# Split order in an expert's first tile: both hidden halves ahead of the next expert's weight blocks

## The chip, the cores and the metric

One core of one Trainium2 chip runs the whole program in one launch. The metric is the device time in microseconds of that core, as the median over executions. TensorE is PE in the rows, with its weight loads as PEld; VectorE is DVE, ScalarE is ACT, GpSimd is POOL and SyncE is SP.

## The reference, cut to what matters

Three stages in a row: attention with pooled queries, a gated mixer, and a mixture of eight experts. The change is in the third one. For every token, one expert `e` is chosen:

```
h = np.maximum(x[b, s] @ w1[e], 0.0)      # 512 -> 1024
out[b, s] = p[e] * (h @ w2[e])            # 1024 -> 512
```

There are 4 x 576 = 2304 tokens. The products are to be exact to about single precision.

## The kernel before, in words

The first two stages end with the tokens sorted by expert in DRAM (`sorted_dram`) and a small table of counts. Function `experts` (line 1376) then works through the experts that have tokens, one after the other, in tiles of 128 tokens. In this run six experts are in use, with 2, 7, 1, 5, 5 and 2 tiles, 22 in all. They are called e0 to e5 here, and the tiles g0 to g21; the first tiles of e0 to e4 are g0, g2, g9, g10 and g15. The numbers of tiles are read by the engines at run time.

Every fp32 product is made of three passes over a high and a low part: ACT rounds a block to its high part (a copy to `F32R`), and DVE or POOL subtracts it from the original to have the low part. This is what "split" means below. It is done for activations and for weights.

One tile on PE (lines 1571 to 1587):

- `first(par, 0, ...)`: 12 matmuls, columns 0 to 511 of the first product into `first_ps[0]`; then 4 matmuls of the second half into `first_ps[1]`.
- `turn_h(g, 0)`: four transposes of the first half of `hidden` into `ht_ps[0]`. They wait for `relu_a`, the ReLU on ACT (L1653).
- the other 8 matmuls of `first(par, 1, ...)`.
- a wait for `ht_lo`, then 6 matmuls of `second` (L1556), `turn_h(g, 1)` (which waits for `relu_b`, the ReLU on DVE, L1724), 6 more, and `turn_x(g + 1)`: four transposes of the next tile's rows into `xt_ps` (L1533), which wait for the rows' DMA.
- a second wait for `ht_lo`, and the last 12 matmuls of `second`. The next tile begins with a wait for `xt_lo`.

ACT rounds `ht_ps[0]`, `ht_ps[1]` (`h_high`, L1609) and `xt_ps` (`x_high`, L1605). DVE makes the low parts (`h_low`, L1679; `x_low`, L1672), and then, for the tile's end, `index` (L1732), `result` (L1734, from `second_ps`) and the next tile's `tag` (L1685). POOL stores `result` by an indirect DMA (L1510).

In an expert's first tile the same engines also split the next expert's weights. w1 has four pieces: ACT rounds them (L1619), DVE subtracts (L1692). w2 has four pieces: ACT rounds them (L1625), POOL subtracts (L1477). Nothing schedules this but the order of the program: each engine has one stream, and `tile` on ACT (line 1651) and on DVE (line 1720) has `split(...)` written between the steps of the tile. Weights of the expert after that are loaded by DMA when their buffer is free: w1 from ACT's queue (L1629), w2 in two halves from POOL's (L1486). An expert's first matmul waits for all four `w1_lo` pieces (line 1569).

Before the change, in an expert's first tile, ACT runs: ReLU, `h_high(g, 0)`, three pieces of w1, `h_high(g, 1)`, `x_high(g + 1)`, the fourth piece of w1, four pieces of w2, and then the ReLU of the second tile. DVE runs: `h_low(g, 0)`, ReLU, one piece, `h_low(g, 1)`, `x_low(g + 1)`, one piece, `index`, `result`, `tag`, the last two pieces, and then the `h_low(g, 0)` of the second tile.

Of the kernel before, what the change touches and what calls it, by code (L numbers as in the profile page):

```python
# [1375 lines left out]
def experts(nc, ctx, sorted_dram, counts, consts, w1, w2, out, stage, first_loaded, first_mark):  # L1376
# [55 lines left out]
    def entry(eng, what, place):  # L1432
        return eng.value_load(counts[0:1, bass.ds(place + what * LIST, 1)], min_val=0, max_val=LIMITS[what])  # L1433
# [8 lines left out]
    with nc.Block() as block:  # L1442
# [147 lines left out]
        def tiles(eng, n, before, tile, split, next_in_use):  # L1590

            with eng.If(n > 0):
                tile(before, next_in_use)
                with eng.If(n > 1):
                    with eng.Fori(1, n) as i:
                        tile(before + i, None)
            with eng.If(n < 1):
                with eng.If(next_in_use > 0):
                    split(range(2 * PIECES))

        @block.scalar
        def _(act):
            def x_high(g):
                act.wait_ge(s["x_turned"], g + 2)
                nc.scalar.copy(xt_h[:].rearrange("p k r -> p (k r)"), xt_ps[:]).then_inc(s["xt_hi"], 1)  # L1605

            def h_high(g, half):
                act.wait_ge(s["h_turned"], 2 * g + half + 1)
                nc.scalar.copy(ht_h[:, 4 * half:4 * half + 4].rearrange("p k r -> p (k r)"), ht_ps[half][:]  # L1609
                               ).then_inc(s["ht_hi"], 1)  # L1610

            def high(e, j, par, pieces):

                for piece in pieces:
                    k = piece % PIECES
                    if piece < PIECES:
                        if k == 0:
                            act.wait_ge(w1_loaded[par], 16 * (j + 1))
                        nc.scalar.copy(w1_h[par][:, k], w1_raw[par][:, k]).then_inc(s["w1_hi"], 1)  # L1619
                    else:  # L1620
                        if isinstance(e, int):
                            act.wait_ge(piece_loaded[k], 16)
                        elif k % 2 == 0:
                            act.wait_ge(half_loaded[k // 2], 16 * e)
                        nc.scalar.copy(w2_h[par][:, 2 * k:2 * k + 2], w2_raw[:, 2 * k:2 * k + 2]  # L1625
                                       ).then_inc(s["w2_hi"], 1)

            def load1(e, par):
                act.dma_start(w1_raw[par], w1_d[entry(act, EXPERT, e)]).then_inc(w1_loaded[par], 16)  # L1629

            high(0, 0, 0, range(PIECES))
            for k in range(PIECES):
                act.dma_start(w2_raw[:, 2 * k:2 * k + 2], w2_d[0][:, 2 * k:2 * k + 2]
                              ).then_inc(piece_loaded[k], 16)
            x_high(0)
            high(0, 0, 0, range(PIECES, 2 * PIECES))
            with act.If(entry(act, IN_USE, 1) > 0):
                load1(1, 1)

            def place(j, par):  # L1640
                e = 2 * j + par
                with act.If(entry(act, IN_USE, e + 2) > 0):
                    act.wait_ge(s["w1_lo"], PIECES * e + PIECES)
                    load1(e + 2, par)
                n, before = (entry(act, what, e) for what in (TILES, BEFORE))
                next_in_use = entry(act, IN_USE, e + 1)

                def split(pieces):
                    high(e + 1, j + par, 1 - par, pieces)

                def tile(g, splits):
                    act.wait_ge(s["first_done"], 2 * g + 1)
                    nc.scalar.activation(hidden[:, 0:FHALF], first_ps[0][:], ACT.Relu).then_inc(s["relu_a"], 1)  # L1653
                    h_high(g, 0)
                    if splits is not None:
                        with act.If(splits > 0):
                            split(range(3))
                    h_high(g, 1)
                    x_high(g + 1)
                    if splits is not None:  # L1660
                        with act.If(splits > 0):
                            split(range(3, 2 * PIECES))

                tiles(act, n, before, tile, split, next_in_use)

            places(act, place)

        @block.vector
        def _(dve):
            def x_low(g):  # L1670
                dve.wait_ge(s["xt_hi"], g + 1)
                nc.vector.tensor_tensor(xt_l[:].rearrange("p k r -> p (k r)"), xt_ps[:],  # L1672
                                        xt_h[:].rearrange("p k r -> p (k r)").bitcast(F32), ALU.subtract
                                        ).then_inc(s["xt_lo"], 1)

            def h_low(g, half):
                part = slice(4 * half, 4 * half + 4)
                dve.wait_ge(s["ht_hi"], 2 * g + half + 1)
                nc.vector.tensor_tensor(ht_l[:, part].rearrange("p k r -> p (k r)"), ht_ps[half][:],  # L1679
                                        ht_h[:, part].rearrange("p k r -> p (k r)").bitcast(F32), ALU.subtract  # L1680
                                        ).then_inc(s["ht_lo"], 1)

            def take_tag(g):
                dve.wait_ge(s["rows_loaded"], 16 * (g + 1))
                nc.vector.tensor_copy(tag[:], rows_in[:, DM:ROW]).then_inc(s["tag_taken"], 1)  # L1685

            def low(e, par, pieces):

                for k in pieces:
                    if k < PIECES:  # L1690
                        dve.wait_ge(s["w1_hi"], PIECES * e + k + 1)
                        nc.vector.tensor_tensor(w1_l[par][:, k], w1_raw[par][:, k],  # L1692
                                                w1_h[par][:, k].bitcast(F32), ALU.subtract
                                                ).then_inc(s["w1_lo"], 1)


            dve.sem_inc(s["tag_taken"], 1)
            dve.sem_inc(s["result_ready"], 1)
            low(0, 0, range(PIECES))
            take_tag(0)  # L1700
            x_low(0)
            for k in range(PIECES):
                part = slice(2 * k, 2 * k + 2)
                dve.wait_ge(s["w2_hi"], k + 1)
                nc.vector.tensor_tensor(w2_l[0][:, part], w2_raw[:, part], w2_h[0][:, part].bitcast(F32),
                                        ALU.subtract).then_inc(s["w2_lo"], 1)

            def place(j, par):
                e = 2 * j + par
                n, before = (entry(dve, what, e) for what in (TILES, BEFORE))  # L1710
                next_in_use = entry(dve, IN_USE, e + 1)

                def split(pieces):
                    low(e + 1, 1 - par, pieces)

                def maybe_split(splits, pieces):
                    if splits is not None:
                        with dve.If(splits > 0):
                            split(pieces)

                def tile(g, splits):
                    h_low(g, 0)
                    dve.wait_ge(s["first_done"], 2 * g + 2)
                    nc.vector.tensor_scalar(hidden[:, FHALF:F2], first_ps[1][:], 0.0, None, ALU.max  # L1724
                                            ).then_inc(s["relu_b"], 1)
                    maybe_split(splits, range(1))
                    h_low(g, 1)
                    x_low(g + 1)
                    maybe_split(splits, range(1, 2))
                    dve.wait_ge(s["tag_taken"], g + 2)  # L1730
                    dve.wait_ge(s["stored"], 16 * g + 16)
                    nc.vector.tensor_copy(index[:], tag[:, 1:2].bitcast(U32)).then_inc(s["result_ready"], 1)  # L1732
                    dve.wait_ge(s["second_done"], g + 1)
                    nc.vector.tensor_scalar(result[:], second_ps[:], tag[:, 0:1], None, ALU.mult  # L1734
                                            ).then_inc(s["result_ready"], 1)
                    dve.wait_ge(s["result_ready"], 2 * g + 3)
                    take_tag(g + 1)
                    maybe_split(splits, range(2, PIECES))

                tiles(dve, n, before, tile, split, next_in_use)  # L1740

            places(dve, place)
# [43 lines left out]
```

## Time and profile before

| | before |
|---|---|
| median of 3 runs | 1269.45 us (1269.32 to 1272.0) |
| the profiled execution, its own time | 1270.8 us |
| its span in the trace | 1269.1 us |
| mean granted clock of TensorE | 0.959 |
| busy: PE, DVE, ACT, POOL | 1172.0, 785.4, 567.6, 537.0 us |
| busy share: PE, DVE, ACT, POOL | 92%, 62%, 45%, 42% |

The experts run from about 952 us to the end. An ordinary tile there takes 12.50 us, in which PE never stops; first tiles and the tiles behind them take longer. A timeline row gives the start in us from the span's start, the duration in us, and in brackets how long the engine had been idle before, with what released it. The start and the duration of neighbouring rows may overlap a little, since an engine begins an instruction before the last one has drained: ACT's casts of 128x1024 last 1.05 us each but follow each other every 0.95 us.

### The profile page before, as it was taken

How to read it: one execution, taken by the hardware profiler on the slowest of the kernel's cores; microseconds unless marked ns; L12 is line 12 of the kernel's file. 1: busy time of each engine (PE TensorE's matmuls, PEld its weight loads, DVE VectorE, ACT ScalarE, POOL GpSimd, SP SyncE). 2: the span in 40 equal slices, each digit the busy share in tenths (PEclk: the TensorE clock that was granted, in tenths of full speed). 3: DMA queues.
4: the chain of work that ended last, by engine and by line, in shares of the span. 5: the costliest groups of instructions: out<-in, count | busy, mean ns of one | idle time of the engine just before them, and what ended most of it. 6: DMA issues, size and time to landing. Idle time of an engine off the chain costs nothing. (4 is left out here: it accounts for less than half of the span.)

```text
span 1269.1 us, 23908 instructions
## 1 busy us (share of the span) xinstructions
PE 1172.0 (92%) x7459; PEld 1053.0 (83%) x7460; DVE 785.4 (62%) x1501; ACT 567.6 (45%) x1022; POOL 537.0 (42%) x597
## 2 busy tenths in 40 slices
PE   6999999999999999997889999999825999799997
PEld 5999999999999999996777989889714778577786
DVE  4888988888888888986532643526134532453532
ACT  4666666666666666663412223222105411341411
POOL 6777777777777777753100010100111520350400
PEclk9999999999999999998899999999856999899999
DMA  5121221212121221101301020120137531350110
GB/s 193 40 65 56 65 65 46 65 56 65 37 65 56 65 65 48 45 9 52 118 1 38 1 75 0 37 83 0 37 104 282 173 108 50 114 203 33 42 33 30
DMA packets 49579, 86.40 MB, mean 68 GB/s; under 512 B 8142, under 2 KB 20558, under 8 KB 49552
## 3 DMA queue, kind: packets, MB, share of 16 engines
q1 hardware_dynamic: 39264, 52.49, 13.2%
q0 software_dynamic: 5984, 19.95, 4.7%
q10 hardware_dynamic: 4304, 13.64, 3.0%
q8 instruction: 13, 0.21, 0.1%
q14 instruction: 14, 0.11, 0.0%
HBM read 69.77 MB, written 17.33 MB: 69 GB/s over the span
## 5 line engine op out<-in xcount | busy, mean ns | idle before, releaser
L618 DVE TENSOR_SCALAR_CACHE_REDUCE probs<-scores 128x1152 f32<-128x1152 f32 x144 | 195.5, 1358 | 61.0 <-PE scores L472 60.0
L472 PE MATMUL scores<-k_t,q_t 128*128 128x384 f32 x960 | 201.7, 347 | 1.3 <-DVE probs L618 1.3
L570 ACT ACTIVATE probs<-probs,neg_max 128x1152 f32<-128x1152 f32 x144 | 181.8, 1263 | 0.0
L594 ACT CAST pt_h<-ring 128x384 fp32r<-128x384 f32 x288 | 139.0, 483 | 73.6 <-PE ring L479 67.8
L495 PE MATMUL acc<-pt_h,v_parts 128*128 128x256 f32 (+1 forms) x576 | 169.3, 316 | 0.6 <-DVE pt_l L684 0.6
L479 PE MATMUL ring<-consts,probs 128*128 128x128 f32 x1296 | 165.4, 273 | 0.7 <-DVE pt_l L684 0.7
L472 PEld LDWEIGHTS scores<-k_t,q_t 128*128 128x128 f32 x960 | 160.7, 189 | 2.2 <-DVE probs L618 2.1
L495 PE MATMUL acc<-pt_l,v_parts 128*128 128x256 f32 (+1 forms) x576 | 157.2, 295 | 0.0
L328 POOL TENSOR_TENSOR pt_l<-mid,pt_h 128x384 fp32r<-128x384 f32 x144 | 145.5, 1010 | 12.0
L479 PEld LDWEIGHTS ring<-consts,probs 128*128 128x128 f32 x1296 | 146.2, 141 | 2.5 <-DVE pt_l L684 1.8
L684 DVE TENSOR_TENSOR pt_l<-ring,pt_h 128x384 fp32r<-128x384 f32 x288 | 145.8, 548 | 0.0
L863 POOL DMA_INDIRECT sorted_tokens<-y,slot x20 | 19.2, 962 | 294.0 <-DVE y L1311 289.1
L325 POOL TENSOR_SCALAR pt_h<-mid 128x384 fp32r<-128x384 f32 x144 | 74.2, 515 | 131.7 <-DVE mid L681 129.9
L495 PEld LDWEIGHTS acc<-pt_h,v_parts 128*128 128x128 f32 x576 | 108.6, 189 | 0.9 <-ACT out_t L577 0.8
L495 PEld LDWEIGHTS acc<-pt_l,v_parts 128*128 128x128 f32 x576 | 109.1, 189 | 0.0
L1679 DVE TENSOR_TENSOR ht_l<-ht_ps,ht_h 128x512 fp32r<-128x512 f32 x44 | 30.4, 691 | 108.1 <-ACT ht_h L1609 108.1
L1510 POOL DMA_INDIRECT out<-result,index x22 | 23.2, 1053 | 159.5 <-DVE result L1734 158.1
L1548 PE MATMUL first_ps<-w_h,xt_h 128*128 128x512 f32 x176 | 72.2, 410 | 10.3 <-DVE w_l L1692 7.0
L681 DVE COPY mid<-ring 128x384 f32<-128x384 f32 x144 | 79.6, 553 | 1.8 <-PE ring L479 1.8
L1556 PE MATMUL second_ps<-w_h,ht_h 128*128 128x512 f32 x176 | 74.0, 421 | 5.9 <-DVE ht_l L1679 5.9
L1548 PE MATMUL first_ps<-w_l,xt_h 128*128 128x512 f32 x176 | 72.9, 414 | 0.0
L1477 POOL TENSOR_TENSOR w_l<-w_raw,w_h 128x1024 fp32r<-128x1024 f32 x20 | 51.7, 2613 | 48.6 <-ACT w_h L1625 48.5
(195 smaller groups left out, 2530.3 us busy)
## 6 DMA issues: line engine op xcount, KB each, us to landing
w_raw<-moe_w POOLq DMA_DIRECT2D x10, 1024.0 KB, 6.2
k_nat<-k SPq DMA_DIRECT2D x32, 288.0 KB, 2.8
v_nat<-v SPq DMA_DIRECT2D x32, 288.0 KB, 2.8
q_nat<-q SPq DMA_DIRECT2D x32, 256.0 KB, 2.9
w_raw<-moe_w ACTq DMA_DIRECT2D x3, 2048.0 KB, 11.0
rows_in<-sorted_tokens SPq DMA_DIRECT2D x23, 257.0 KB, 2.6
x_in<-x_heads SPq DMA_DIRECT2D x18, 256.0 KB, 3.3
x_heads<-x_pair SPq DMA_DIRECT2D x16, 256.0 KB, 2.4
```

The costliest lines, as they stand in the source:

```text
L325: nc.gpsimd.tensor_scalar(out, src, 1.0, 1.0, ALU.mult, ALU.mult).then_inc(signal, 1)
L328: nc.gpsimd.tensor_tensor(out, src, high_part.bitcast(F32), ALU.subtract).then_inc(signal, 1)
L472: mm = nc.tensor.matmul(scores[:, c, 0:CK], q_t[par][:, side, t * P:(t + 1) * P], k_t[par][:, c * CK:(c + 1) * CK], start=(i == 0), stop=( ...
L479: mm = nc.tensor.transpose(ring[c][:, i * P:(i + 1) * P], probs[n % 3][:, c, i * P:(i + 1) * P], ident)
L495: mm = nc.tensor.matmul(acc[:, 0:b - a], v_parts[par][:, kt], part[:, kt, a:b], start=(kt == 0 and part is pt_h), stop=(kt == KT - 1 and p ...
L570: nc.scalar.activation(probs[n % 3][:], probs[n % 3][:], ACT.Exp, bias=neg_max[:, n % 3:n % 3 + 1], scale=-1.0, accum_out=row_sum[:, n:n + ...
L594: nc.scalar.copy(pt_h[:, 3 * c:3 * c + 3, n * P:(n + 1) * P], ring[c][:, 0:CK].rearrange("p (i r) -> p i r", i=3)).then_inc(s["high_done"], 1)
L618: nc.vector.tensor_scalar(probs[n % 3][:], scores[:, :, 0:CK], -0.5 * DH ** -0.5, None, ALU.mult, ALU.min, accum_out=neg_max[:, n % 3:n % ...
L681: nc.vector.tensor_copy(mid[n % 3][:], ring[1][:, 0:CK]).then_inc(s["mid_done"], 1)
L684: nc.vector.tensor_tensor(pt_l[:, 3 * c:3 * c + 3, cols], ring[c][:, 0:CK].rearrange("p (i r) -> p i r", i=3), pt_h[:, 3 * c:3 * c + 3, co ...
L1548: mm = nc.tensor.matmul(first_ps[half][:], a[:, k], w[:, k, cols], start=(i == 0), stop=(i == 3 * KD - 1))
L1556: mm = nc.tensor.matmul(second_ps[:], a[:, k], w[:, k], start=(k == 0 and n == 0), stop=(k == K2 - 1 and n == 2))
```

## The change

In `tile`, ACT's `h_high(g, 1)` is moved ahead of `split(range(3))`, and DVE's `h_low(g, 1)` ahead of `split(range(1))`. In tiles without a split nothing differs.

```diff
@@ scalar, tile @@
                     h_high(g, 0)
+                    h_high(g, 1)
                     if splits is not None:
                         with act.If(splits > 0):
                             split(range(3))
-                    h_high(g, 1)
                     x_high(g + 1)
@@ vector, tile @@
+                    h_low(g, 1)
                     maybe_split(splits, range(1))
-                    h_low(g, 1)
                     x_low(g + 1)
```

ACT, an expert's first tile, from the ReLU on (L1653 the ReLU, L1609 `h_high`, L1619 the pieces of w1 of the next expert, L1605 `x_high`):

```order
 L1653 ACTIVATE hidden<-first_ps 128x512
 L1609 CAST ht_h<-ht_ps 128x512
-L1656 COMPARE_AND_BRANCH
+L1608 REGISTER_ALU
+L1609 CAST ht_h<-ht_ps 128x512
+L1657 COMPARE_AND_BRANCH
 L1618 ISA
 L1619 CAST w_h<-w_raw 128x1024 x3
-L1656 UNCONDITIONAL_BRANCH
-L1608 REGISTER_ALU
-L1609 CAST ht_h<-ht_ps 128x512
```

The second cast of `ht_ps` with its wait now stands ahead of three casts of weights instead of behind them.

DVE, the same tile, from its ReLU on (L1724 the ReLU, L1679 `h_low`, L1692 a piece of w1's low part, L1672 `x_low`):

```order
 L1724 TENSOR_SCALAR hidden<-first_ps 128x512
+L1679 TENSOR_TENSOR ht_l<-ht_ps,ht_h 128x512
 L1718 COMPARE_AND_BRANCH
 L1691 ISA
 L1692 TENSOR_TENSOR w_l<-w_raw,w_h 128x1024
 L1718 UNCONDITIONAL_BRANCH
-L1679 TENSOR_TENSOR ht_l<-ht_ps,ht_h 128x512
 L1671 REGISTER_ALU
 L1672 TENSOR_TENSOR xt_l<-xt_ps,xt_h 128x512
```

The second subtraction now stands ahead of the one piece of weights instead of behind it. The streams of PE, POOL and SP are the same as before, with their DMAs, and no instruction is added or taken away on any engine.

## Rows read from the trace of the kernel before

**Rows 1.** Waits from 950 us to the end: total us, times, longest us.
```profile
PE second_ps L1556 <- DVE ht_l L1679: 5.9, 4, 1.9
PE first_ps L1548 <- DVE w_l L1692: 7.0, 1, 7.0
```
**Rows 2.** Timeline of ACT, e3's first tile: start, us, what, [idle before].
```profile
1112.28 0.59 ACT L1609 CAST ht_h<-ht_ps 128x512 fp32r<-128x512 f32 x1 [0.77 <-PE ht_ps L1540]
1112.77 2.94 ACT L1619 CAST w_h<-stage 128x1024 fp32r<-128x1024 f32 x3
1115.98 0.59 ACT L1609 CAST ht_h<-ht_ps 128x512 fp32r<-128x512 f32 x1 [0.27 <-PE ht_ps L1540]
1117.81 0.59 ACT L1605 CAST xt_h<-xt_ps 128x512 fp32r<-128x512 f32 x1 [1.25 <-PE xt_ps L1533]
...
1121.40 2.00 ACT L1625 CAST w_h<-w_raw 128x1024 fp32r<-128x1024 f32 x2 [0.16 <-DMA w_raw<-moe_w]
1123.41 0.60 ACT L1653 ACTIVATE hidden<-first_ps 128x512 f32<-128x512 f32 x1
```
**Rows 3.** Timeline of DVE, e3's first tile from `x_low` to the second tile's `h_low`.
```profile
1118.43 0.69 DVE L1672 TENSOR_TENSOR xt_l<-xt_ps,xt_h 128x512 fp32r<-128x512 f32 x1 [1.14 <-ACT xt_h L1605]
1119.04 1.22 DVE L1692 TENSOR_TENSOR w_l<-stage,w_h 128x1024 fp32r<-128x1024 f32 x1
...
1120.62 0.75 DVE L1734 TENSOR_SCALAR result<-second_ps,tag 128x512 f32<-128x512 f32 x1 [0.30 <-PE second_ps L1556]
1121.49 1.33 DVE L1685 COPY tag<-rows_in 128x2 f32<-128x2 f32 x1
1122.74 4.55 DVE L1692 TENSOR_TENSOR w_l<-stage,w_h 128x1024 fp32r<-128x1024 f32 x2
1127.21 0.68 DVE L1679 TENSOR_TENSOR ht_l<-ht_ps,ht_h 128x512 fp32r<-128x512 f32 x1
```
**Rows 4.** Timeline of POOL, the same stretch.
```profile
1120.38 5.83 POOL L1477 TENSOR_TENSOR w_l<-w_raw,w_h 128x1024 fp32r<-128x1024 f32 x2 [6.30 <-ACT w_h L1625]
```
**Rows 5.** Timeline of PE, e3's second tile: three of its rows.
```profile
1120.41 0.40 PE L1548 MATMUL first_ps<-w_h,xt_h 128*128 128x512 f32 x1
...
1124.14 0.60 PE L1540 MATMUL ht_ps<-consts,hidden 128*128 128x128 f32 x4
...
1127.94 0.50 PE L1556 MATMUL second_ps<-w_h,ht_h 128*128 128x512 f32 x1 [1.33 <-DVE ht_l L1679]
```
**Rows 6.** Timeline of ACT, e1's first tile: `h_high(g, 1)` and `x_high`.
```profile
1003.85 0.59 ACT L1609 CAST ht_h<-ht_ps 128x512 fp32r<-128x512 f32 x1 [0.27 <-PE ht_ps L1540]
1006.70 0.59 ACT L1605 CAST xt_h<-xt_ps 128x512 fp32r<-128x512 f32 x1 [2.27 <-PE xt_ps L1533]
```
**Rows 7.** Timeline of ACT, e0's two tiles.
```profile
974.35 2.94 ACT L1619 CAST w_h<-w_raw 128x1024 fp32r<-128x1024 f32 x3 [2.63 <-DMA w_raw<-moe_w]
977.20 0.57 ACT L1609 CAST ht_h<-ht_ps 128x512 fp32r<-128x512 f32 x1
...
982.92 2.00 ACT L1625 CAST w_h<-w_raw 128x1024 fp32r<-128x1024 f32 x2 [1.82 <-DMA w_raw<-moe_w]
985.99 0.60 ACT L1653 ACTIVATE hidden<-first_ps 128x512 f32<-128x512 f32 x1 [1.06 <-PE first_ps L1548]
```
**Rows 8.** Timeline of PE, e0: transposes, the matmul that waited, the second tile's first.
```profile
974.20 0.60 PE L1540 MATMUL ht_ps<-consts,hidden 128*128 128x128 f32 x4
...
978.55 0.50 PE L1556 MATMUL second_ps<-w_h,ht_h 128*128 128x512 f32 x1 [1.93 <-DVE ht_l L1679]
...
982.76 0.63 PE L1548 MATMUL first_ps<-w_h,xt_h 128*128 128x512 f32 x1
```
**Rows 9.** PE by stretches: length, PE busy (matmuls), granted clock, DMA share, GB/s.
```profile
980.00:983.00 3.00, 3.00 (x8) 0.50 0.64 246
...
1015.00:1018.00 3.00, 1.67 (x8) 1.00 0.24 19
...
1106.30:1109.60 3.30, 3.22 (x8) 0.50 0.70 199
```

## Prediction

> **What bounds the kernel now.** I read the waits of the experts' stage first, then the timelines of ACT, DVE, POOL and PE around one first tile, then the granted clock. The waits show that PE sets the pace: in the last 319 us it waits for a low part of `hidden` four times, 5.9 us in all, and once for a low part of w1, 7.0 us [rows 1]. The four are 1.93 us in e0's first tile [rows 8] and 1.33 us in the second tile of e1, e3 and e4, of which one is shown [rows 5]. So the question for each of the five first tiles (g0, g2, g9, g10, g15) is whether the second half of `hidden` is what PE waits for, and what the moved step pushes back.
>
> It is what PE waits for in e0 only. There three weight casts had waited for their DMA until 974.35, and the cast of `ht_ps[1]` came at 977.20 [rows 7], though its transposes, begun at 974.20, last 0.60 us [rows 8]. In the other four the three casts fit into the time in which ACT would wait for the transposes anyway: in e3 they run from 1112.77 to 1115.71, ACT is then idle for 0.27 us, and the cast of `ht_ps[1]` starts at 1115.98, when PE is ready [rows 2]. e1 shows the same 0.27 [rows 6]. The move takes nothing from these.
>
> **The change, step by step, in e3's first tile.** With the new order ACT stands still from the end of its first cast (1112.87) to 1115.98. The three weight casts follow that cast: they start 0.48 us behind it (as 1112.77 behind 1112.28, rows 2) at 1116.46 and take 3 x 0.95, so `xt_h` starts at 1119.31. Before, it started at 1117.81: 1.50 us later. The fourth w1 cast and the first w2 cast follow at once in both orders, so they are 1.50 later too. This is the price of the edit: 2.85 us of weight casts moved out of a cover of 3.1 us into a place where 1.25 us of idle time [rows 2] was free.
>
> Who waits for that. (a) PE's next tile needs `xt_lo`: DVE starts 0.62 behind ACT and takes 0.69, so 1119.31 + 1.31 = 1120.62, against PE's start at 1120.41 [rows 5]: some 0.25 us, not lasting, since a later wait is longer. (b) The ReLU of the second tile stands behind the w2 casts. 1119.31 + 0.48 + 0.95 + 4 x 0.95 = 1124.54 instead of 1123.41, 1.13 later, and PE's transposes follow it directly [rows 2, 5]. (c) DVE: `x_low`, the second piece and `index` are 1.50 later. `result` had 0.30 us of idle time before it [rows 3], so it is 1.20 later. (d) POOL's first subtraction waits for ACT's first w2 cast, so it goes from 1120.38 to 1121.88, 1.50 later [rows 4].
>
> DVE's last two weight pieces decide, since the second tile's `ht_l` stands behind them, and PE had already waited 1.33 us for it: no slack is left there. Alone a piece takes 1.22 us (the row at 1119.04); beside POOL two take 4.55, and the tag copy ended 2.44 us behind POOL's start (1121.49 + 1.33 against 1120.38) [rows 3, 4]. e1's and e4's do so too. I read it as DVE and POOL taking turns, so that the chain hangs on POOL's start, and take 1.50 us for e3; without that link it would be 1.20. The Trainium skill, "SBUF — State Buffer", says of the port pair that DVE and GpSimd share that it is an exclusive lock held for the whole instruction, the other one fully blocked. By that rule each such shift is 1.50 us and the sum for e2, e3 and e4 is 4.5 us; if the two only slowed each other down, it would be 3.6.
>
> The other tiles. **e4** is e3 again: +1.50. **e2** has one tile, and PE waits 7.0 us for the last w1 piece [rows 1], which is the same chain on DVE: +1.50. **e1**: the rows of the next tile came late, ACT had 2.27 us of idle time before `x_high` [rows 6], and 1003.85 + 0.48 + 2.85 = 1007.18 is only 0.48 behind 1006.70: +0.48.
>
> **e0** gains. The cast of `ht_ps[1]` can start at about 974.84, `ht_l` ends 1.31 later at 976.15, and PE, whose idle time began at 978.55 - 1.93 = 976.62 [rows 8], goes on without it. `xt_h` then starts at 974.84 + 0.48 + 2.85 = 978.17, 0.49 later than before; PE's second tile can start at about 979.55, 3.2 us earlier than the 982.76 of before [rows 8]. But its transposes of `hidden` wait for a ReLU that stands behind two w2 casts on ACT, which waited for their DMA until 982.92 [rows 7]. The DMA's issue does not move. They end at 984.92, so the ReLU gains 985.99 - 984.9 = 1.1 us and no more. PE, ahead by then, waits some 2.2 us for it.
>
> The clock comes in here. Before, it was at 0.50 of full speed (the 1.2 GHz level) in the 3 us from 980 on, right behind the idle 1.93 us, while in the stretch of e1's 1.33 us, from 1015 to 1018, it stayed at 1.00 [rows 9]. A fall cost some eight matmuls (x8 in 3.0 us, rows 9) of about 0.427 us instead of 0.233 (e3's twelve and four from 1120.41 to 1124.14, rows 5, 3.73 / 16): 1.55 us. The 2.2 us wait is longer than the one that was followed by a fall, so I count one: e0 comes to -1.1 + 1.55 = about +0.4 against this trace. In e0 before, half of the fall was hidden behind the same ReLU.
>
> The second tiles of e1, e3 and e4 then have waits of about 1.6, 1.7 and 1.7 us for `ht_l`, where they had 1.33 (1.33 + 1.50 - 1.13 = 1.70). That lies between the row that kept its clock and the row that lost it. Unknown, so bounded: no fall, 0; a fall in all three, +4.6 us. A gain is excluded, since none of these tiles is at the lower clock now. The middle of the two rows is 1.63, with two waits just above and one at it; I count one fall of three, +1.5. After e2 PE restarts at 0.50 as it does now [rows 9] for a few us; I take no difference, with a bound of +0.7 and -0.7 (about half of a fall).
>
> Nothing is issued more or less. SP's row loads wait for `tag`, and move with it by up to 1.5 us, but the transposes that need them come a tile later. POOL's stores and w2 loads move with their chain.
>
> **Sum.** 0.48 + 3 x 1.50 + 0.4 + 1.5 = 6.9 us. Against the profiled execution's own 1270.8 that is 1277.7. The median of the three runs, 1269.45, lies 1.35 below it, so I set the forecast at 1269.45 + 6.9 = **1276.4 us**, 0.54% slower.
>
> **The rivals.**
>
> *The clock holds everywhere in the second tiles.* The sum is 5.4 with e0's fall, 3.9 without: 1273.3 to 1274.9. For it speaks that 1.33 us of idle time was kept three times of three. It is still slower, and I hold it with the forecast as one mechanism with two sizes: forecast (one or two falls) 0.50, this one 0.26.
>
> *The clock falls in all three second tiles*, and the restart after e2 is longer: 6.9 + 3.1 + 0.7 = 10.7, 1280.2. Each wait alone is below 1.93. Chance 0.12.
>
> *The delay of ACT is mostly free.* If the next rows came as late in e2, e3 and e4 as in e1, each shift would be 0.48 and not 1.50: 4 x 0.48 + 0.4 = 2.3, 1271.8, within the noise. Against it: e3 waits 1.25 us for the transposes themselves and not for a DMA [rows 2]. Chance 0.09.
>
> *Faster: only e0 counts.* If ACT's queue went past the waiting cast to the weight casts behind it, the order of the program would not matter in e1 to e4, and e0 would keep its 1.1 us: 1268.3, and with the clock's fall avoided and the DMA earlier by more than 2 us, up to 3.2: 1266.2. It decides from the point where `xt_h` in e2 to e4 is late by less than 0.2 us. Against it: ACT's rows stand in program order everywhere, and in e0 the cast of `ht_ps[1]` did wait behind casts that waited for a DMA [rows 7]. Chance 0.03.
>
> **How the numbers follow.** A measurement of this kernel can tell about 0.2%, 2.5 us, from no change. The two clock sizes and the full fall are slower by more than that: 0.50 + 0.26 + 0.12 = 0.88. The mostly free case is the same, 0.09, and the last one faster, 0.03. The range goes from 1272.4, the case with no fall at all less the 0.9 us by which DVE's shifts may be smaller, to 1280.2, the full fall. It leaves out the last two cases, 0.12, and what lies beyond the bounds.
>
> **What would show it.** ACT's cast of `ht_ps[1]` directly behind the first one in the row order, with 3.1 us of idle time before it in e1 to e4; `xt_h` 3.33 us behind the moved cast instead of 1.83; POOL's first subtraction and `ht_l` of the second tile both 1.5 us later against PE's first transposes; PE's wait before it 1.6 to 1.7 us plus some 0.8 us before the transposes; PE's wait in front of e3 8.5 us instead of 7.0; no wait for `ht_l` in e0's first tile, but one of about 2.2 us before the second tile's transposes. I am wrong if PE's second tiles of e3 and e4 start their `second` matmuls by less than 1 us later, or if e0 gains more than 1.5 us.

## The result, and the profile after

| | before | after |
|---|---|---|
| median | 1269.48 us (1264.08 to 1272.0, 12 runs) | 1276.46 us (1273.23 to 1278.67, 12 runs) |
| the profiled execution, its own time | 1270.8 us | 1276.51 us |
| its span | 1269.1 us | 1274.9 us |
| mean granted clock | 0.959 | 0.957 |

The ratio is 1.0056, with a 95% interval of 1.0043 to 1.0069: the change makes the kernel 7.0 us slower (5.5 to 8.8). The two profiled executions differ by 5.7 us in their own times.

Waits from 950 us to the end, after (total us, times, longest us):

```profile
PE first_ps L1548 <- DVE w_l L1692: 8.4, 1, 8.4
PE second_ps L1556 <- DVE ht_l L1679: 5.2, 3, 1.7
PE ht_ps L1540 <- ACT hidden L1653: 3.4, 4, 1.9
```

Against [rows 1]: of the four waits for a low part of `hidden`, e0's of 1.93 us is gone, and the three others grew from 1.33 to 1.73. The wait in front of e3 grew from 7.0 to 8.4. The third row is new against this trace of before. PE waits for the ReLU four times: 1.85 us in e0's second tile, and 0.50 in those of e1, e3 and e4.

ACT in e3's first tile, after (answers to [rows 2]):

```profile
1114.96 0.58 ACT L1609 CAST ht_h<-ht_ps 128x512 fp32r<-128x512 f32 x1 [0.77 <-PE ht_ps L1540]
1118.66 0.58 ACT L1609 CAST ht_h<-ht_ps 128x512 fp32r<-128x512 f32 x1 [3.12 <-PE ht_ps L1540]
1119.15 2.95 ACT L1619 CAST w_h<-stage 128x1024 fp32r<-128x1024 f32 x3
1122.00 0.58 ACT L1605 CAST xt_h<-xt_ps 128x512 fp32r<-128x512 f32 x1
1122.47 1.05 ACT L1619 CAST w_h<-stage 128x1024 fp32r<-128x1024 f32 x1
1123.42 3.89 ACT L1625 CAST w_h<-w_raw 128x1024 fp32r<-128x1024 f32 x4
1127.22 0.59 ACT L1653 ACTIVATE hidden<-first_ps 128x512 f32<-128x512 f32 x1
```

From one cast of `ht_ps` to the other ACT does nothing for 3.12 us, and the idle time before `xt_h` is gone. `xt_h` starts 1122.00 - 1118.66 = 3.34 us behind the moved cast, where it was 1.83. The ReLU starts 8.56 us behind it, where it was 7.43.

DVE, the same stretch, after (answers to [rows 3]):

```profile
1122.61 0.69 DVE L1672 TENSOR_TENSOR xt_l<-xt_ps,xt_h 128x512 fp32r<-128x512 f32 x1 [1.15 <-ACT xt_h L1605]
1123.22 1.21 DVE L1692 TENSOR_TENSOR w_l<-stage,w_h 128x1024 fp32r<-128x1024 f32 x1
...
1124.42 0.74 DVE L1734 TENSOR_SCALAR result<-second_ps,tag 128x512 f32<-128x512 f32 x1
1125.28 1.70 DVE L1685 COPY tag<-rows_in 128x2 f32<-128x2 f32 x1
1126.90 4.55 DVE L1692 TENSOR_TENSOR w_l<-stage,w_h 128x1024 fp32r<-128x1024 f32 x2
1131.37 0.68 DVE L1679 TENSOR_TENSOR ht_l<-ht_ps,ht_h 128x512 fp32r<-128x512 f32 x1
```

POOL, after (answers to [rows 4]):

```profile
1124.55 5.81 POOL L1477 TENSOR_TENSOR w_l<-w_raw,w_h 128x1024 fp32r<-128x1024 f32 x2 [8.38 <-ACT w_h L1625]
```

PE in e3's second tile, after (answers to [rows 5]):

```profile
1123.36 0.50 PE L1548 MATMUL first_ps<-w_h,xt_h 128*128 128x512 f32 x1
...
1127.86 0.65 PE L1540 MATMUL ht_ps<-consts,hidden 128*128 128x128 f32 x4 [0.50 <-ACT hidden L1653]
1132.10 0.50 PE L1556 MATMUL second_ps<-w_h,ht_h 128*128 128x512 f32 x1 [1.73 <-DVE ht_l L1679]
```

Taken from the moved cast, POOL's first subtraction starts at 5.89, where it was 1120.38 - 1115.98 = 4.40: 1.49 later. `result` is 1.12 later (5.76 against 4.64), yet the second tile's `ht_l` is 1.48 later (12.71 against 11.23). So DVE lost 0.36 us more between the two rows. The difference sits in the tag copy, which took 1.70 us where it took 1.33. It ended 1126.98 - 1124.55 = 2.43 us behind POOL's start; before it was 2.44. DVE reached the copy earlier against POOL and was let in no sooner.

e0, ACT after (answers to [rows 7]):

```profile
974.68 0.58 ACT L1609 CAST ht_h<-ht_ps 128x512 fp32r<-128x512 f32 x1 [3.12 <-PE ht_ps L1540]
...
982.68 1.99 ACT L1625 CAST w_h<-w_raw 128x1024 fp32r<-128x1024 f32 x2 [1.25 <-DMA w_raw<-moe_w]
984.58 0.59 ACT L1653 ACTIVATE hidden<-first_ps 128x512 f32<-128x512 f32 x1
```

and PE after (answers to [rows 8]):

```profile
985.23 0.66 PE L1540 MATMUL ht_ps<-consts,hidden 128*128 128x128 f32 x4 [1.85 <-ACT hidden L1653]
```

PE by stretches, after (length, PE busy, granted clock, DMA share, GB/s; answers to [rows 9]):

```profile
980.00:983.00 3.00, 3.00 (x15) 1.00 0.42 160
986.80:990.00 3.20, 3.20 (x9) 0.50 0.41 101
1130.00:1133.00 3.00, 1.27 (x6) 1.00 0.28 18
```

The fall of the clock moved from behind the wait at 976.6 to behind the one at 983.4. In e3's second tile 1.73 us of waiting left it at full speed.

So that traces can be compared, I use the ReLU's starts (L1653), from an expert's first tile to its third, and for e2 from its one tile to e3's first:

| us | e0 | e1 | e2 | e3 | e4 |
|---|---|---|---|---|---|
| before, first trace | 29.02 | 27.63 | 21.22 | 26.61 | 26.61 |
| after, first trace | 29.44 | 28.09 | 23.27 | 28.09 | 28.10 |
| difference | +0.42 | +0.46 | +2.05 | +1.48 | +1.49 |

The differences sum to 5.9 us, which is all that the two spans differ by (5.8).

### The profile page after: what moved, and what is told of

Its sections match the earlier page's. It is cut to its first block and busy times, and to the rows that moved or that the text cites. A ratio compares the mean times of both kernels' runs of the same rounds, so it can differ in the third digit from the quotient of the medians.

```text
span 1274.9 us, 23908 instructions
## 1 busy us (share of the span) xinstructions
PE 1174.4 (92%) x7459; PEld 1053.0 (83%) x7460; DVE 788.9 (62%) x1501; ACT 566.3 (44%) x1022; POOL 537.0 (42%) x597
## 5 line engine op out<-in xcount | busy, mean ns | idle before, releaser
L325 POOL TENSOR_SCALAR pt_h<-mid 128x384 fp32r<-128x384 f32 x144 | 74.0, 514 | 132.4 <-DVE mid L681 130.7
L1679 DVE TENSOR_TENSOR ht_l<-ht_ps,ht_h 128x512 fp32r<-128x512 f32 x44 | 30.3, 690 | 114.0 <-ACT ht_h L1609 114.0
```

The costliest lines, as they stand in the source:

```text
L325: nc.gpsimd.tensor_scalar(out, src, 1.0, 1.0, ALU.mult, ALU.mult).then_inc(signal, 1)
```

## The experiments

Each was made from the kernel before. "Ratio" is to that kernel, run on the same chip.

**ACT's half of the change alone.**

```diff
@@ scalar, tile @@
                     h_high(g, 0)
+                    h_high(g, 1)
                     if splits is not None:
                         with act.If(splits > 0):
                             split(range(3))
-                    h_high(g, 1)
```

> ACT's part of the change alone, DVE as before. My theory (the price is ACT's three weight casts moved behind the transposes' wait, and the chain xt_h, POOL's first subtraction, DVE's last two pieces): e2, e3 and e4 cost 1.5 us each and e1 0.5, as with the whole change. In e0 to e4 DVE's first piece now waits for ACT's first weight cast ahead of the second half's low part, so PE gets a new wait of about 1.6 us in the first tiles of e1, e3 and e4, but it lies beside the later wait for DVE's chain and costs nothing on top. e0 comes to between -1.1 and +0.4. Sum +3.9 to +5.4 us: ratio 1.003 to 1.0045. Rival (DVE's part carries the cost): within 0.1% of before.

Measured: 1276.16 us, ratio 1.005 (1.0037 to 1.0063). In its profiled execution e3 takes 28.09 us and e4 28.09, as with the whole change, and e2 22.92. The expected new wait is there, on DVE's first piece and on PE:

```profile
1120.67 1.23 DVE L1692 TENSOR_TENSOR w_l<-stage,w_h 128x1024 fp32r<-128x1024 f32 x1 [2.71 <-ACT w_h L1619]
1121.82 0.68 DVE L1679 TENSOR_TENSOR ht_l<-ht_ps,ht_h 128x512 fp32r<-128x512 f32 x1
```

and in PE's waits from 966 us on it shows as seven where the kernel before had four:

```profile
PE second_ps L1556 <- DVE ht_l L1679: 8.6, 7, 1.6
```

In e3 and e4 PE waits 1.65 us for `ht_l` in the first tile and 0.91 in the second. With the whole change it waits 0.50 for the ReLU and 1.73 for `ht_l`, both in the second tile. From ReLU to ReLU the stretch is the same. So ACT's half carries the cost, and DVE's half only decides in which tile PE stands still. In e1's first tile the expected wait did not come, because PE stood still for late rows there (below). The sum is above what I had expected (6.3 us against 3.9 to 5.4), and e1 took 29.21. There PE waited 1.95 us for the next rows, and PE's first matmul behind that took 0.78 us, where the same one takes 0.48 at full clock:

```profile
1007.01 1.02 PE L1533 MATMUL xt_ps<-consts,rows_in 128*128 128x128 f32 x4 [1.95 <-DMA rows_in<-sorted_tokens]
1007.69 0.78 PE L1556 MATMUL second_ps<-w_h,ht_h 128*128 128x512 f32 x1
```

This run also shows how the tag copy hangs on POOL. In e3 DVE came to the copy 1.53 us behind POOL's start, later than in either kernel of the case, and the copy was shorter by as much. It again ended 2.44 us behind that start:

```profile
1125.00 5.82 POOL L1477 TENSOR_TENSOR w_l<-w_raw,w_h 128x1024 fp32r<-128x1024 f32 x2 [8.00 <-ACT w_h L1625]
1126.53 0.91 DVE L1685 COPY tag<-rows_in 128x2 f32<-128x2 f32 x1
```

**DVE's half alone.**

```diff
@@ vector, tile @@
+                    h_low(g, 1)
                     maybe_split(splits, range(1))
-                    h_low(g, 1)
```

> DVE's part of the change alone, ACT as before. My theory: the second half's low part waits for ACT either way, the first piece goes from the idle time before it into the 1.14 us of idle time before x_low, so at most 0.1 us per first tile; ratio 0.9995 to 1.0005. Rival (the cost of the change sits on DVE: the piece behind h_low pushes x_low and all that follows): +1.2 us in each of e1 to e4, ratio 1.004.

Measured: 1271.08 us, ratio 1.0009 (0.9999 to 1.002). e3 26.61, e4 26.59, PE's wait in front of e3 7.0, all as before. e1 took 28.44, with a wait of 1.64 us for late rows. The rival, 1.004, is out. The median itself is a little above what I expected and its interval takes in no change.

**The new order in e0 alone.**

```diff
@@ scalar, tile @@
                     if splits is not None:
                         with act.If(splits > 0):
-                            split(range(3))
+                            with act.If(before > 0):
+                                split(range(3))
                     h_high(g, 1)
+                    if splits is not None:
+                        with act.If(splits > 0):
+                            with act.If(before < 1):
+                                split(range(3))
```

with DVE's half as in the last experiment.

> ACT's new order in e0's first tile alone (a branch on the number of tiles before), DVE's new order everywhere. My theory: PE's wait of 1.9 us in e0's first tile goes and one of about 2 us before the second tile's transposes comes, since the ReLU stands behind two casts that wait for their DMA; between -1.1 us (clock not lowered) and +0.4 us (lowered behind that wait), so ratio 0.9990 to 1.0005. Rival (the removed wait and its clock are a real gain of 3 us, given back elsewhere by the rest of the change): ratio 0.9975. The other rival (the whole change's cost comes from e0): ratio 1.005.

Measured: 1270.75 us, ratio 1.0008 (0.9999 to 1.0017). A gain of 3 us is out, and so is a cost of 5. e1 to e4 lie within what the kernel before shows in its traces (27.13, 21.63, 26.61 and 26.60). e0 took 28.48 us with the new wait in its place, and here, behind 1.76 us, the clock did not fall. PE's waits from 966 us on:

```profile
PE second_ps L1556 <- DVE ht_l L1684: 4.4, 4, 1.3
PE ht_ps L1540 <- ACT hidden L1653: 1.8, 1, 1.8
```

**The dose: one weight cast ahead of `h_high(g, 1)`, two behind it.**

```diff
                         with act.If(splits > 0):
-                            split(range(3))
+                            split(range(1))
                     h_high(g, 1)
+                    if splits is not None:
+                        with act.If(splits > 0):
+                            split(range(1, 3))
```

> A dose between the two orders: one of ACT's three weight casts ahead of h_high(g, 1), two behind it; DVE as before. My theory (ACT has 1.25 us of idle time before x_high, two casts of 0.95 and the 0.48 of the cast itself take 2.38): x_high 0.55 us later in e2, e3 and e4, nothing in e1, e0 -1.1. Sum 3 x 0.55 - 1.1 = +0.5 us, ratio 0.9995 to 1.0015, and POOL's first subtraction 0.55 us later in the timeline. Rival (any cast behind the wait costs its own 0.95): two of them, +1.9 in each of four, ratio 1.005.

Measured: 1272.42 us, ratio 1.0022 (1.0011 to 1.0034). ACT in e3's first tile:

```profile
1116.89 0.59 ACT L1609 CAST ht_h<-ht_ps 128x512 fp32r<-128x512 f32 x1 [2.16 <-PE ht_ps L1540]
1117.37 2.00 ACT L1619 CAST w_h<-stage 128x1024 fp32r<-128x1024 f32 x2
1119.27 0.58 ACT L1605 CAST xt_h<-xt_ps 128x512 fp32r<-128x512 f32 x1
```

and POOL:

```profile
1121.84 5.81 POOL L1477 TENSOR_TENSOR w_l<-w_raw,w_h 128x1024 fp32r<-128x1024 f32 x2 [7.59 <-ACT w_h L1625]
```

and DVE's `result` and the second tile's `ht_l`:

```profile
1121.69 0.74 DVE L1737 TENSOR_SCALAR result<-second_ps,tag 128x512 f32<-128x512 f32 x1
...
1128.66 0.68 DVE L1682 TENSOR_TENSOR ht_l<-ht_ps,ht_h 128x512 fp32r<-128x512 f32 x1
```

`xt_h` is 2.38 us behind the cast, 0.55 later than before, and POOL's start is 4.95 behind it, 0.55 later. e3 and e4 took 27.15 each, +0.54. That is the expected step, not 1.9. The median is above my sum (1.0005 expected at the middle), and the interval leaves that middle out. In the profiled execution the five stretches sum to 131.5 us, where the three traces of the kernel before have 131.1, 132.4 and 130.1. Its first ReLU started at 971.32 us, 1.4 to 1.8 us later than theirs and ahead of the first edited place. Whether that holds for the median too is not shown.

**The dose: two ahead, one behind.** The same edit with `range(2)` and `range(2, 3)`.

> The other end of the dose: two of ACT's three weight casts ahead of h_high(g, 1), one behind it; DVE as before. My theory: behind the cast (0.48) one weight cast (0.95) fits, 1.43 against the 1.83 us at which x_high started before, so e1 to e4 take what they take before (26.6 us from the first tile's ReLU to the third's in e3 and e4); e0 gains up to 1.4 us, since its second half waits for two casts and not three. Ratio 0.9988 to 1.0. Rival (each cast behind the wait costs its own time): +0.95 in each of four, ratio 1.003.

Measured: 1270.55 us, ratio 1.0007 (0.9994 to 1.002). e3 26.59 and e4 26.60. The rival, 1.003, is out. A gain from e0 does not show in the median. So with three, two, one and none of the casts ahead of the wait, e4 takes 26.61, 26.60, 27.15 and 28.10 us: the first cast behind it is free, the second costs 0.55, the third 0.95.

**One w1 piece more ahead on DVE.** ACT as before.

```diff
@@ vector, tile @@
-                    maybe_split(splits, range(1))
+                    maybe_split(splits, range(2))
                     h_low(g, 1)
                     x_low(g + 1)
-                    maybe_split(splits, range(1, 2))
+                    maybe_split(splits, range(2, 3))
...
-                    maybe_split(splits, range(2, PIECES))
+                    maybe_split(splits, range(3, PIECES))
```

> ACT as before; DVE moves one piece of w1 forward: two ahead of h_low(g, 1), one behind x_low, and one, not two, in front of the second tile's h_low. It tests that DVE's last pieces are what PE waits for in the second tiles. My theory: the low part of the second half is 0.4 us later, just in time for PE; the 1.33 us waits in the second tiles of e1, e3 and e4 go, -1.33 each; in front of e3 the w1 wait of 7.0 us falls to about 3.7, but PE then waits for POOL's last w2 piece inside e3's first tile, so -0.5 to -1 there. Sum -4.5 to -5, ratio 0.9960 to 0.9967. Rival (the second tile's ReLU on ACT, which stood 0 to 0.3 us behind its casts, is the real bound): -0.3 us each, ratio 0.999.

Measured: 1265.56 us, ratio 0.9969 (0.9958 to 0.998). PE's waits from 966 us on:

```profile
PE first_ps L1548 <- DVE w_l L1692: 3.5, 1, 3.5
PE first_ps L1548 <- POOL w_l L1477: 2.4, 1, 2.4
...
PE second_ps L1556 <- DVE ht_l L1679: 1.1, 1, 1.1
```

The three waits of 1.33 us are gone (the 1.1 is e0's), and e4 takes 25.26 us, 1.35 less. The wait in front of e3 fell by 3.5 us, and 2.4 of that came back as a wait for POOL's w2 piece inside e3's first tile, so that e2 and e3 together take 47.25 us instead of 47.83. The gain is 4.1 us, a little less than the 4.5 to 5 that I expected. DVE's last pieces are what PE's second tiles wait for, and the ReLU is not the bound in the order of before.

**Both orders together**, two ahead on each engine:

> The two kernels before together: on ACT two of the three weight casts ahead of h_high(g, 1), on DVE two pieces ahead of h_low(g, 1). My theory: the gains add, -4.5 to -5 from DVE's order and 0 to -1.4 from e0, ratio 0.995 to 0.9965. Rival (DVE's two pieces and ACT's later third cast get in each other's way, and PE waits for the second half's low part in each first tile): ratio 0.998 or above.

Measured: 1263.27 us, ratio 0.9948 (0.9928 to 0.9967), faster than both kernels of the case. The gain of 6.4 us is slightly more than I had expected at most (0.995), and the rival, 0.998, is out. e4 takes 25.26 us, and PE waits nowhere for a low part of `hidden`.

**Both kernels again, for their traces.** No edit.

> The changed kernel once more, for its trace. Open: whether its 1.73 us waits in the second tiles of e1, e3 and e4 ever lower the clock (my forecast counted one fall of three, 1.5 us), or whether the rest between the profiles' difference (5.7 us) and the medians' (7.0) lies in e0 and behind the restart after e2. If the first: 29.6 us instead of 28.1 from ReLU to ReLU in one of e3, e4. If the second: 28.1 in both, and e0 or the stretch around e2 moves by 0.5 to 1.5 us from one trace to the next.

> A second trace of the changed kernel on the same chip: 28.1 us in e3 and e4 if 1.73 us of waiting keeps the clock, 29.6 where it does not; e0 between 28.5 and 29.5, the stretch around e2 22.7 or 23.3.

> The kernel before once more, for its trace: the same question from the other side. If e0 carries the rest, e0 takes 27.5 to 28.5 us here (ReLU of the first tile to ReLU of the third) where the first profile had 29.02.

> A second trace of the kernel before on the same chip: 26.6 us in e3 and e4, e0 27.5 to 29.0 by when its weights land and whether the clock falls behind the wait for them, the stretch around e2 21.2 to 22.2.

| us | own time | e0 | e1 | e2 | e3 | e4 |
|---|---|---|---|---|---|---|
| after, again | 1279.20 | 29.58 | 28.12 | 23.09 | 28.10 | 28.09 |
| after, again | 1278.76 | 30.21 | 28.10 | 22.68 | 28.09 | 28.10 |
| before, again | 1272.33 | 29.94 | 26.75 | 22.15 | 26.97 | 26.61 |
| before, again | 1269.66 | 28.18 | 26.60 | 22.15 | 26.60 | 26.60 |

The second of the two possibilities holds: the difference lies elsewhere than in the second tiles. In nine second tiles of the new order (three traces of e1, e3, e4) PE waited 1.72 to 1.75 us for `ht_l`, and in none did the clock fall. One of these waits and the longer one in e0, in the second of the new traces (columns as above):

```profile
985.40:988.00 2.60, 0.00 (x0) 1.00 0.38 101
988.30:991.50 3.20, 3.20 (x11) 0.50 0.27 28
...
1132.70:1134.30 1.60, 0.00 (x0) 1.00 0.00 0
```

What varies is e0 (28.18 to 29.94 before, 29.44 to 30.21 after), the restart behind e2, and, before the change, e1. In the second of the old traces ACT's rows in e1's first tile are those of e3:

```profile
1002.84 0.59 ACT L1609 CAST ht_h<-ht_ps 128x512 fp32r<-128x512 f32 x1 [0.27 <-PE ht_ps L1540]
1004.68 0.59 ACT L1605 CAST xt_h<-xt_ps 128x512 fp32r<-128x512 f32 x1 [1.26 <-PE xt_ps L1533]
```

The 2.27 us of idle time in [rows 6] had been a row load that came late in that execution.

## Why the prediction was right, and where not

The forecast was 1276.4 us, the measured median 1276.46. That it is so close is luck, since two terms were off in opposite directions. The main mechanism is right: casts moved out of a wait delay POOL, and with POOL the weight pieces that PE waits for.

- **e3 and e4, 1.50 each.** Measured +1.48 and +1.49 in the first pair of traces. By steps: `xt_h` 3.34 us behind the moved cast (3.33 foreseen), the ReLU 1.13 later (1.13), POOL 1.49 later (1.50), PE's wait 1.73 (1.70). The second tile's transposes of `hidden` start 4.50 us behind its first matmul, where it was 3.73: 0.77 later (some 0.8 foreseen), of which the view of waits shows 0.50, as a matmul's record (0.40 us) overlaps the next one's, which begins 0.23 us behind it. Right. ACT's half alone, and the dose, show the cause.
- **DVE hangs on POOL's start**, so 1.50 and not 1.20. The tag copy ended 2.43 us behind POOL's start in the new order and 2.44 in the old one, while DVE arrived at it at another distance. The run with ACT's half alone adds a third distance (1.53) with the same end (2.44). The run with one cast ahead tells the two sizes apart: `result` was 0.16 us later (4.80 behind the cast against 4.64), POOL 0.55 later, and the second tile's `ht_l` 0.54 later (11.77 against 11.23). It moved with POOL's start and not with DVE's own arrival. The Trainium skill's "SBUF — State Buffer", section "Who interferes with whom", says that when a DVE and a GpSimd instruction both need the port pair which the two engines share, the one issued first holds it to its end and the other is fully blocked. The copy's end, 2.43 to 2.44 us behind POOL's start whenever DVE came, agrees.
- **e2, 1.50.** PE's wait grew from 7.02 to 8.45, 1.43. The stretch grew by 2.05 in the first pair: the clock stayed low for longer, 10.2 us instead of 6.8. With three traces on each side, the mean is 23.01 against 21.84, +1.2. The old order has both lengths too, for the same 7.0 us wait, so the extra 0.6 of the first pair is not the change's.
- **e1, 0.48.** This term was mis-sized. It fitted the first pair (+0.46), but rested on [rows 6], a late row load that neither of the other two old traces has at such length. Means of three: 28.10 against 26.99, +1.1. Where the rows come in time, e1 costs 1.5 like the others.
- **e0, +0.4.** Measured +0.42 in the first pair; means of three 29.74 against 29.05, +0.7. As foreseen, PE waits 1.85 to 2.73 us for a ReLU behind a DMA, with the clock's fall behind it in all three new traces, and alone the new order in e0 gives no gain (ratio 1.0008). But the wait that the term took away, 1.93 us, belongs to the first trace. In the two repeats of the kernel before the three weight casts began at 972.66 and 972.75, not at 974.35, PE waited there for nothing and for 0.41 us, and it already had the wait for the ReLU (2.41 us with a fall of the clock, 1.72 without one). So the size of this term rests on when weights landed in one execution, and that it fitted is luck.
- **One clock fall in the second tiles, +1.5.** This step failed. I had placed the wait between a row that kept its clock (1.33 us) and one that lost it (1.93), and counted one of three. Nine of nine kept it at 1.72 to 1.75 us.

Means of three traces give 0.70 + 1.11 + 1.17 + 1.37 + 1.49 = 5.8 us for the experts' stage. That lies inside the 5.5 to 8.8 us of the timed runs. The rest to the median's 7.0, if it is one, I cannot place: the first tile's ReLU itself starts between 969.48 and 972.20 us in the three new traces and between 969.59 and 969.94 in the old ones, ahead of anything that the change touches. In the two late ones the stage's first transposes had waited for the rows' DMA until 963.34 and 962.93, in the four others until 960.60 to 961.42.

Of the rivals, the one in which the clock holds in the second tiles had the mechanism right, at 1273.3 to 1274.9. With e1 at its usual size and e0's fall it would have been 1275.9. The other three are out: the clock fell in none of the three second tiles, the delay was not free, and ACT did stand still behind its waiting cast.

## What to carry to other kernels

In an in-order stream, ready work is free in front of a step with a wait as long as it fits into that wait: here three casts (2.85 us) had filled a 3.1 us gap, and putting the waiting step first turned the gap into idle time and the casts into delay. Behind the step only so much is free as there is idle time before the next one that matters, here one cast of the three. What is late is found by asking what ended the idle time before it: the moved cast had been waiting for its producer (0.27 us) in four of five first tiles, so moving it up could not bring it forward. And what had been the last wait (DVE's final weight pieces in the second tile) is where an edit of the same kind paid.

## What the runs showed of the hardware that I had not expected

- The granted clock, in this stage, from the point where it had come to full speed (969.6 us in the first trace): PE waits of up to 1.76 us left it there in all traces, those of 1.85, 1.93, 1.95, 2.15, 2.36, 2.41, 2.43 and 2.73 us were each followed by 3.4 us at half speed.
- In the same wait of 7.0 us in front of e3 the clock fell while PE stood still, and it was low for 6.8 us in three traces (21.2 to 21.6 us for the stretch) and for 10.2 in three others (22.15).
- A DVE copy of 128x2 elements takes 0.17 us alone, and 0.91, 1.33 or 1.70 beside POOL's subtraction: in e3 it ended 2.43 to 2.44 us behind POOL's start, though DVE came to it 1.53, 1.11 or 0.73 us behind that start.
